# Turning the gates behind the scores in a gated linear attention kernel

## The chip, the cores and the metric

The kernel runs on one core of one Trainium2 chip. The metric is device time in microseconds (us), from inputs in HBM to the output in HBM; lower is better. Engines are named as the profile names them: PE is TensorE (PEld its weight loads), DVE is VectorE, ACT is ScalarE, POOL is GpSimd, SP is SyncE, which here only issues DMAs.

## The reference, cut to what matters

Attention with a gated state, then a routed expert network, then a dense network. Only the first part is touched by the change:

```
q, k, v, f_logit: (4, 8, 768, 48)          # batch, heads, sequence, head dimension
f = 1 / (1 + exp(-f_logit))
for t in range(S):
    state = f[:, :, t, :, None] * state + einsum('bhd,bhe->bhde', k[:, :, t], v[:, :, t])
    y[:, :, t] = einsum('bhd,bhde->bhe', q[:, :, t], state)
x = y as (3072, 384)
x = expert network of x: 8 experts, 384 -> 1024 -> 384, 384 tokens each, chosen by sorted logits
out = (h * clip(h + 3, 0, 6) / 6) @ w_out,  h = x @ w_in,  384 -> 2048 -> 384
```

## The kernel before

Each engine has its own program, and semaphores order them. Attention is cut into 24 units: 6 tiles of 128 positions times 4 batches (NT = 24, B = 4). A unit has all 8 heads of one batch in one tile, as 4 pairs of heads. `units` (L443) writes units 0 to 3 out, puts 4 to 19 into a loop whose body holds four units (so n is a register expression there), and writes 20 to 23 out. The first unit of a loop body is therefore 4, 8, 12 or 16.

The inputs come with positions on the partitions, and the products need head dimensions there, so TensorE turns them against the identity: `turn_f`, `turn_k`, `turn_q` (L1394 on), each four transposes of 128x128 recorded at L1392. It works ahead: in unit n it turns f and k of unit n + 2 and q of unit n + 1. The rest of a unit on TensorE, in this order: the scores (L1448, k_sc by q_sc, 16 passes in tiles of 64x128), the turn of the scaled k called kn (L1459, in all but the last four units), the turns of k and q, `turn_y` of the unit before (L1431, 128x128), the state's part of y (L1475, 64x64), the products of k and v for the state (L1484, 128x64), and the values (L1491, 128x48). The last unit's turn_y stands behind all units.

What the turn of f starts is a chain over three engines:
- ScalarE: `exp(n + 2)` (L792, e_x from the turned f; waits for f_turned), then den (L796).
- VectorE: `products(n + 2)` (L999), a scan over den that gives grow. It waits for den_done, then for ln_done, error_done (up to 2n - 1) and k_scaled.
- ScalarE: `decays(n + 2)`, lnr (L802) and guess (L806).
- GpSimd: `refine(n + 2)` of its unit n: error (L688), error again (L691), decay (L696), then last_decay (L683), and behind it w_low of the weight chunk (L708), a subtraction in which both inputs lie in SBUF.
- VectorE: `scale_k(n + 2)` (L1005) needs grow; `scale_q(n + 1)` (L1010) needs decay of n + 1.

VectorE's order in a unit is the mask of the scores (L1048, two instructions), the scan, scale_k, scale_q, kv_sum (L1067), the logits (L1015), the state (L1073). ScalarE's is exp, den, the copy of kn (L836), the copies of x (L817, L820), lnr, guess, the cast of a weight chunk (L827), the copy of y (L845). The scores of unit n + 1 need q_sc of n + 1, which is VectorE's scale_q in unit n.

SP issues the loads of f, k, q and v four units ahead into four buffers each (the load of f(n) waits until f(n - 4) is turned), and with each unit one store of x and one load of a weight chunk, in one queue.

Unit 0 has seven matmuls of filling (`busy`) behind its turn of f, before the scores.

Of the kernel before, what the change touches and what calls it, by code (L numbers as in the profile page):

```python
# [15 lines left out]
B, H, S, D = 4, 8, 768, 48  # L16
# [41 lines left out]
def build(nc, q, k, v, f, wg, w1, w2, wi, wo, out):  # L58
    ctx = ExitStack()
    with ctx:  # L60
# [392 lines left out]
        def start_of(n):  # L453

            return n if isinstance(n, int) else NT

        def more_state(tt):

            return not isinstance(tt, int) or tt < TT - 1
# [925 lines left out]
        def _(pe):  # L1385
# [3 lines left out]
            def turn(n, tt, b, src, dst, here, done):  # L1389
                pe.wait_ge(here[b], 16 * (tt + 1))  # L1390
                for g in range(PAIRS):
                    last = pe.transpose(dst[:, P * g:P * g + P], src[:, b, 2 * g:2 * g + 2, :].rearrange("p a b -> p (a b)"), ident[:, :])  # L1392
                last.then_inc(done, 1)

            def turn_f(n, tt, b):
                if start_of(n) >= 1:
                    pe.wait_ge(exp_done, n)
                turn(n, tt, b, f_in, fT_ps, loaded_f, f_turned)

            def turn_k(n, tt, b):  # L1400
                if start_of(n) >= 1:
                    pe.wait_ge(k_scaled, n)
                turn(n, tt, b, k_in, kT_ps, loaded_k, k_turned)

            def turn_q(n, tt, b):
                if start_of(n) >= 1:
                    pe.wait_ge(q_scaled, n)
                turn(n, tt, b, q_in, qT_ps, loaded_q, q_turned)

            def busy(count):  # L1410
                for i in range(count):
                    pe.matmul(p4[:, P * (i % 4):P * (i % 4) + P], ident[:, :], ident[:, :], start=True, stop=True)
# [9 lines left out]
            def turn_y(n, i):  # L1422
                pe.wait_ge(yT_copied, n + 1)
                if start_of(n) >= 1:
                    pe.wait_ge(x_copied, n)
                else:
                    pe.wait_ge(loaded_wg, 48)
                    pe.wait_ge(turn_made, 2)
                pe.sem_inc(passed, 1)
                for g in range(PAIRS):  # L1430
                    last = pe.matmul(x_ps[:, g, :], yT[:, i, P * g:P * g + P], turn_gate[:, g, :], start=True, stop=True)  # L1431
                last.then_inc(x_ready, 1)

            def unit(n, tt, b, more):
                i = b % 2
                if more:
                    turn_f(n + 2, tt + b // 2, (b + 2) % B)
                if isinstance(n, int) and n == 0:
                    busy(BUSY[2])
                pe.wait_ge(q_scaled, n + 1)  # L1440
                pe.wait_ge(k_scaled, n + 1)
                if start_of(n) >= 1:
                    pe.wait_ge(masked, n)
                pe.sem_inc(passed, 1)
                for g in range(PAIRS):
                    for j in range(2):
                        r = slice(HALF * j, HALF * j + HALF)
                        last = pe.matmul(a_ps[j][:, P * g:P * g + P], k_sc[r, i, P * g:P * g + P], q_sc[r, i, P * g:P * g + P],  # L1448
                                         start=True, stop=True)
                last.then_inc(a_ready, 1)  # L1450
                if not more_state(tt) and b == B - 1:
                    pe.wait_ge(steep_rows, 1)
                    pe.wait_ge(exp_done, NT)
                    pe.matmul(p0[:, 0:1], ones[:, :], steep_sum[:, :], start=True, stop=True).then_inc(steep_summed, 1)
                if more_state(tt):
                    if start_of(n) >= 1:
                        pe.wait_ge(kv_added, n)
                    for g in range(PAIRS):
                        last = pe.transpose(kn_ps[:, P * g:P * g + P], k_sc[:, i, P * g:P * g + P], ident[:, :])  # L1459
                    last.then_inc(kn_ready, 1)  # L1460
                if more:
                    turn_k(n + 2, tt + b // 2, (b + 2) % B)
                if more or b < B - 1:
                    turn_q(n + 1, tt + (b + 1) // B, (b + 1) % B)
                if start_of(n) >= 1:
                    turn_y(n - 1, 1 - i)
                if start_of(n) >= B:
                    pe.wait_ge(state_done, n - B + 1)
                if start_of(n) >= 1:
                    pe.wait_ge(yT_copied, n)  # L1470
                pe.sem_inc(passed, 1)
                for h in range(H):
                    g, j = h // 2, h % 2
                    r = slice(HALF * j, HALF * j + HALF)
                    last = pe.matmul(yT_ps[r, P * g:P * g + P], state[r, b, g, :], q_sc[r, i, P * g:P * g + P],  # L1475
                                     start=(g == 0), stop=False, skip_group_check=True)
                last.then_inc(y_init, 1)
                pe.wait_ge(loaded_v[b], 16 * (tt + 1))
                if more_state(tt):
                    pe.wait_ge(kn_copied, n + 1)  # L1480
                    pe.sem_inc(passed, 1)
                    for h in range(H):
                        g, j = h // 2, h % 2
                        last = pe.matmul(kv_ps[HALF * j:HALF * j + HALF, g, :], kn[:, P * g + HALF * j:P * g + HALF * j + HALF],  # L1484
                                         v_in[:, b, h, :], start=True, stop=True)
                    last.then_inc(kv_ready, 1)
                pe.wait_ge(masked, n + 1)
                pe.sem_inc(passed, 1)
                for h in range(H):
                    g, j = h // 2, h % 2  # L1490
                    last = pe.matmul(yT_ps[HALF * j:HALF * j + D, P * g:P * g + P], v_in[:, b, h, :], a_sb[:, i, j, g, :],  # L1491
                                     start=False, stop=(g == PAIRS - 1), skip_group_check=True)
                last.then_inc(y_ready, 1)
            units(pe, unit)
            go = steep_flag(pe)
            turn_y(NT - 1, (B - 1) % 2)
# [305 lines left out]
```

## Time and profile before

| | us |
|---|---|
| median of 3 runs | 829.54 (829.25 to 831.32) |
| the profiled execution | 828.84 |
| its span | 827.1 |
| PE busy in the span | 798.6 (97%) |
| DVE, ACT, POOL busy | 358.1, 318.1, 328.3 |
| mean granted clock of TensorE | 0.992 of full speed |

The first 169 us are attention, then comes the routing to about 207 us, then the experts and the dense network to the end. In slices of a fortieth of the span (20.7 us) PE is at 9 tenths or more from the second to the seventh, and DVE at 8, so that stage has little slack on either; behind it, in the experts' stage, PE alone is full. Below, rows in order of time have the start in us, the duration in us, the engine, the line, what is written from what, the count of instructions, and in brackets how long the engine was idle before and who ended that.

### The profile page before, as it was taken

The numbers are of one execution on the slowest core, as the hardware profiler recorded it, in microseconds if no ns is written. First come the engines' busy times: TensorE is split into PE (matmuls) and PEld (weight loads), VectorE is DVE, ScalarE is ACT, GpSimd is POOL, SyncE is SP. The second block draws the span as 40 slices with busy tenths as digits, with TensorE's granted clock in tenths as the row PEclk, the third lists the DMA queues.
The fourth block names the chain that finished last, engine by engine and source line by source line (L and its number), as shares of the span: only waits on it lengthen the run. The fifth ranks groups of instructions, "written<-read, shape, count | busy, mean of one in ns | idle before, by whom it ended". The sixth has DMA issues, their size and how long they took to land.

```text
span 827.1 us, 15012 instructions
## 1 busy us (share of the span) xinstructions
PE 798.6 (97%) x5785; PEld 762.4 (92%) x5785; DVE 358.1 (43%) x653; ACT 318.1 (38%) x626; POOL 328.3 (40%) x247
## 2 busy tenths in 40 slices
PE   7899999986999999999999999999999999999996
PEld 6788888844999999999999999999999999999996
DVE  7888888655234314422431343144224323431332
ACT  4776667512233314322332333134324323332332
POOL 3778888746144115322602440254216124401001
PEclk9999999998999999999999999999999999999999
DMA  9999999542113012210221040122102210200000
GB/s 153 202 192 184 213 190 191 109 172 97 39 26 128 15 43 77 77 58 0 76 76 57 3 149 0 57 76 76 47 10 76 76 57 0 76 0 29 1 0 29
DMA packets 126801, 64.97 MB, mean 79 GB/s; under 512 B 102448, under 2 KB 119856, under 8 KB 126768
## 3 DMA queue, kind: packets, MB, share of 16 engines
q1 hardware_dynamic: 123696, 55.09, 30.4%
q0 software_dynamic: 3072, 9.44, 3.6%
q8 instruction: 21, 0.34, 0.2%
q14 instruction: 12, 0.10, 0.0%
HBM read 55.07 MB, written 9.44 MB: 78 GB/s over the span
## 4 chain that ended last, share of the span: by engine, by line
PE 90%; DVE 3%; SPq 3%; DMA 2%; issue 1%; ACT 1%; POOL 0%; POOLq 0%; DVEq 0%; ACTq 0%
PE psum L1666 24%; PE psum L1668 24%; PE psum L1667 24%; PE psum L1392 3%; PE psum L1448 3%; PE psum L1475 2%; PE psum L1431 2%; PE psum L1491 2%; SPq L530 2%; PE psum L1459 1%; PE psum L1484 1%; PE psum L1677 1%; PE psum L1575 1%; DMA f_in<-in_f_logit_dram 1%; DMA raw<-in_moe_w_in_dram 1%
## 5 line engine op out<-in xcount | busy, mean ns | idle before, releaser
L1374 DVE SCALAR_TENSOR_TENSOR psum<-rg,psum 128x384 f32<-128x384 f32 x128 | 71.9, 562 | 155.1 <-ACT rg L945 155.1
L945 ACT ACTIVATE rg<-psum,three 128x384 f32<-128x384 f32 x128 | 74.4, 581 | 153.0 <-PE psum L1668 153.0
L1666 PE MATMUL psum<-yh,w_high 128*128 128x384 f32 x384 | 130.6, 340 | 0.8
L1666 PE MATMUL psum<-w_high,gh 128*128 128x384 f32 x384 | 128.4, 334 | 0.3 <-DVE gl L1377 0.3
L1668 PE MATMUL psum<-yh,w_low 128*128 128x384 f32 x384 | 128.4, 334 | 0.0
L1667 PE MATMUL psum<-yl,w_high 128*128 128x384 f32 x384 | 128.4, 334 | 0.0
L1668 PE MATMUL psum<-w_high,gl 128*128 128x384 f32 x384 | 128.3, 334 | 0.0
L1667 PE MATMUL psum<-w_low,gh 128*128 128x384 f32 x384 | 128.3, 334 | 0.0
L781 POOL DMA_INDIRECT out_dram<-ys,ids x24 | 24.0, 999 | 251.2 <-ACT ys L960 246.4
L1364 DVE SCALAR_TENSOR_TENSOR hl<-psum,hh 128x384 fp32r<-128x384 f32 x64 | 35.7, 558 | 164.9 <-ACT hh L935 158.3
L1377 DVE SCALAR_TENSOR_TENSOR gl<-psum,gh 128x384 fp32r<-128x384 f32 x128 | 71.4, 558 | 72.3 <-ACT gh L949 72.3
L949 ACT ACTIVATE gh<-psum 128x384 fp32r<-128x384 f32 x128 | 62.9, 491 | 81.4 <-DVE psum L1374 81.4
L935 ACT ACTIVATE hh<-psum 128x384 fp32r<-128x384 f32 x64 | 31.5, 492 | 144.9 <-PE psum L1668 144.3
L723 POOL CAST w1h<-raw 128x3072 fp32r<-128x3072 f32 (+1 forms) x13 | 22.9, 1764 | 138.6 <-PE psum L1668 128.3
L1666 PEld LDWEIGHTS psum<-yh,w_high 128*128 128x128 f32 x384 | 72.1, 188 | 4.3 <-DVE yl L1368 3.4
L1666 PEld LDWEIGHTS psum<-w_high,gh 128*128 128x128 f32 x384 | 72.1, 188 | 0.6 <-DVE gl L1377 0.6
L1667 PEld LDWEIGHTS psum<-yl,w_high 128*128 128x128 f32 x384 | 72.2, 188 | 0.0
L1668 PEld LDWEIGHTS psum<-yh,w_low 128*128 128x128 f32 x384 | 72.1, 188 | 0.0
L1667 PEld LDWEIGHTS psum<-w_low,gh 128*128 128x128 f32 x384 | 72.1, 188 | 0.0
L1668 PEld LDWEIGHTS psum<-w_high,gl 128*128 128x128 f32 x384 | 72.1, 188 | 0.0
L1666 PE MATMUL psum<-xh,w1h 128*128 128x384 f32 (+2 forms) x198 | 65.8, 332 | 0.5 <-DVE xl L1358 0.2
L1668 PE MATMUL psum<-xh,w1l 128*128 128x384 f32 (+2 forms) x198 | 65.6, 331 | 0.0
(194 smaller groups left out, 1504.7 us busy)
## 6 DMA issues: line engine op xcount, KB each, us to landing
raw<-in_moe_w_dram SPq DMA_DIRECT2D x15, 1536.0 KB, 6.5
f_in<-in_f_logit_dram SPq DMA_DIRECT2D x24, 192.0 KB, 4.7
k_in<-in_k_dram SPq DMA_DIRECT2D x24, 192.0 KB, 5.1
q_in<-in_q_dram SPq DMA_DIRECT2D x24, 192.0 KB, 5.3
v_in<-in_v_dram SPq DMA_DIRECT2D x24, 192.0 KB, 4.7
x_rows<-x_nat SPq DMA_DIRECT2D x24, 192.0 KB, 4.1
raw<-in_moe_w_in_dram SPq DMA_DIRECT2D x12, 256.0 KB, 4.3
raw<-in_moe_w_out_dram SPq DMA_DIRECT2D x12, 256.0 KB, 3.2
```

Source lines behind the costliest of these rows:

```text
L781: pool.indirect_dma_start(out=out[:, :], out_offset=bass.IndirectOffsetOnAxis(ap=ids[:, 3 * e + t:3 * e + t + 1].bitcast(U32), axis=0), in ...
L935: act.activation(hh[:, j % 2, :], banks[j % 2][:, 0:CAP], ACT.Relu).then_inc(hh_done, 1)
L945: act.activation(rg[:, j % 2, :], banks[j % 3][:, 0:CAP], ACT.Relu, bias=three[:, 0:1]).then_inc(r_done, 1)
L949: act.mul(gh[:, j % 3, :], banks[j % 3][:, 0:CAP], 1.0 / 6.0).then_inc(gh_done, 1)
L1364: dve.scalar_tensor_tensor(out=hl[:, j % 2, :], in0=banks[j % 2][:, 0:CAP], scalar=0.0, in1=hh[:, j % 2, :].bitcast(F32), op0=ALU.max, op1 ...
L1374: dve.scalar_tensor_tensor(out=bank, in0=rg[:, j % 2, :], scalar=6.0, in1=bank, op0=ALU.min, op1=ALU.mult).then_inc(gg_done, 1)
L1377: dve.scalar_tensor_tensor(out=gl[:, j % 3, :], in0=bank, scalar=1.0 / 6.0, in1=gh[:, j % 3, :].bitcast(F32), op0=ALU.mult, op1=ALU.subtra ...
L1392: last = pe.transpose(dst[:, P * g:P * g + P], src[:, b, 2 * g:2 * g + 2, :].rearrange("p a b -> p (a b)"), ident[:, :])
L1448: last = pe.matmul(a_ps[j][:, P * g:P * g + P], k_sc[r, i, P * g:P * g + P], q_sc[r, i, P * g:P * g + P], start=True, stop=True)
L1666: pe.matmul(bank, high, rhs_high, start=start, stop=False)
L1667: pe.matmul(bank, high, rhs_low, start=False, stop=False)
L1668: return pe.matmul(bank, low, rhs_high, start=False, stop=stop)
```

## The change

In unit n, for all n but 0, the turn of f of unit n + 2 no longer stands at the head of the unit, between the values of unit n - 1 and the scores of unit n; it stands right behind the scores, ahead of the turns of kn, k and q. In unit 0 (`opening`) it stays where it is, with the filling behind it. The waits go with it: turn_f waits for exp_done of the unit before and for the load of f.

```
             def unit(n, tt, b, more):
                 i = b % 2
-                if more:
-                    turn_f(n + 2, tt + b // 2, (b + 2) % B)
-                if isinstance(n, int) and n == 0:
+                opening = isinstance(n, int) and n == 0
+                if opening:
+                    turn_f(2, 0, 2)
                     busy(BUSY[2])
                 pe.wait_ge(q_scaled, n + 1)
                 pe.wait_ge(k_scaled, n + 1)
...
                 last.then_inc(a_ready, 1)
+                if more and not opening:
+                    turn_f(n + 2, tt + b // 2, (b + 2) % B)
                 if not more_state(tt) and b == B - 1:
```

## Rows read from the trace of the kernel before

**Rows 1.** Busy time of each engine in a stretch; the columns stand in the first line.
```profile
core 0: us, PE busy (x) PEld busy (x) DVE busy (x) ACT busy (x) POOL busy (x), PEclk, DMA share, GB/s
100.00:120.00 20.00, 20.00 (x270) 17.67 (x268) 16.56 (x25) 14.22 (x28) 16.74 (x16) 1.00 1.18 193
```

**Rows 2.** Weight loads of TensorE in order of time, unit 7 and the next f.
```profile
60.53 0.42 PEld L1392 LDWEIGHTS psum<-ident,f_in 128*128 128x128 f32 x4 [0.18 <-issue]
61.12 0.97 PEld L1448 LDWEIGHTS psum<-q_sc,k_sc 64*128 64x128 f32 x16 [0.17 <-issue]
62.21 0.42 PEld L1459 LDWEIGHTS psum<-ident,k_sc 128*128 128x128 f32 x4
62.60 0.47 PEld L1392 LDWEIGHTS psum<-ident,k_in 128*128 128x128 f32 x4
63.03 0.47 PEld L1392 LDWEIGHTS psum<-ident,q_in 128*128 128x128 f32 x4
...
65.56 0.55 PEld L1484 LDWEIGHTS psum<-v_in,kn 128*64 128x64 f32 x16 [0.17 <-issue]
66.02 0.83 PEld L1491 LDWEIGHTS psum<-a_sb,v_in 128*48 128x48 f32 x16
67.04 0.42 PEld L1392 LDWEIGHTS psum<-ident,f_in 128*128 128x128 f32 x4 [0.19 <-issue]
```

**Rows 3.** ScalarE in order of time, unit 7.
```profile
61.23 0.60 ACT L792 ACTIVATE e_x<-psum 128x512 f32<-128x512 f32 x1
61.86 0.63 ACT L796 ACTIVATE den<-e_x 128x512 f32<-128x512 f32 x1
...
65.10 0.64 ACT L802 ACTIVATE lnr<-grow 128x512 f32<-128x512 f32 x1
```

**Rows 4.** VectorE in order of time, unit 7.
```profile
62.33 1.29 DVE L1048 TENSOR_TENSOR a_sb<-psum,causal 128x512 f32<-128x512 f32 x2 [0.95 <-PE psum L1448]
63.53 1.25 DVE L999 TENSOR_TENSOR_SCAN grow<-den,cap 128x516 f32<-128x516 f32 x1
```

**Rows 5.** GpSimd in order of time, unit 7.
```profile
63.68 2.18 POOL L708 TENSOR_TENSOR w_low<-raw,w_high 128x512 f32 x1
66.49 1.18 POOL L688 TENSOR_TENSOR error<-grow,guess 128x512 f32<-128x512 f32 x1 [0.63 <-ACT guess L806]
```

**Rows 6.** Weight loads of TensorE, the turn of f in unit 9.
```profile
73.91 0.42 PEld L1392 LDWEIGHTS psum<-ident,f_in 128*128 128x128 f32 x4 [0.55 <-issue]
```

**Rows 7.** VectorE's q_sc in unit 1 and TensorE's scores in unit 2.
```profile
27.74 0.68 DVE L1010 TENSOR_TENSOR q_sc<-psum,decay 128x512 f32<-128x512 f32 x1
...
28.54 1.00 PEld L1448 LDWEIGHTS psum<-q_sc,k_sc 64*128 64x128 f32 x16 [0.60 <-issue]
```

**Rows 8.** The turns of f in units 20 and 21, and q_sc between.
```profile
145.53 0.42 PEld L1392 LDWEIGHTS psum<-ident,f_in 128*128 128x128 f32 x4 [0.18 <-issue]
...
150.47 0.68 DVE L1010 TENSOR_TENSOR q_sc<-psum,decay 128x512 f32<-128x512 f32 x1
...
151.13 0.42 PEld L1392 LDWEIGHTS psum<-ident,f_in 128*128 128x128 f32 x4 [0.18 <-issue]
```

**Rows 9.** Scores, mask, scan and w_low in order of time, unit 8.
```profile
67.63 1.16 PE L1448 MATMUL psum<-q_sc,k_sc 64*128 64x128 f32 x16
...
68.93 1.29 DVE L1048 TENSOR_TENSOR a_sb<-psum,causal 128x512 f32<-128x512 f32 x2 [1.04 <-PE psum L1448]
...
70.13 1.22 DVE L999 TENSOR_TENSOR_SCAN grow<-den,cap 128x516 f32<-128x516 f32 x1
70.18 2.25 POOL L708 TENSOR_TENSOR w_low<-raw,w_high 128x512 f32 x1
```

**Rows 10.** w_low, scan and q_sc of unit 4, scores of unit 5.
```profile
44.02 1.27 POOL L708 TENSOR_TENSOR w_low<-raw,w_high 128x512 fp32r<-128x512 f32 x1
...
44.11 2.27 DVE L999 TENSOR_TENSOR_SCAN grow<-den,cap 128x516 f32<-128x516 f32 x1
...
47.12 0.68 DVE L1010 TENSOR_TENSOR q_sc<-psum,decay 128x512 f32<-128x512 f32 x1
...
48.10 0.64 PEld L1448 LDWEIGHTS psum<-q_sc,k_sc 64*128 64x128 f32 x10 [0.17 <-issue]
```

## The prediction

> **What bounds the kernel now.** First the busy time by stretch: in attention, where the change is, TensorE is busy 20.00 of 20 us at a granted clock of 1.00; the reader is to see that VectorE (16.6 us) and GpSimd (16.7 us) are near it too [rows 1]. Then TensorE's weight loads in order of time, for one unit (unit 7; units 0 to 23 are the 24 pairs of tile and batch). I count from the start of f's turn: f 0, scores 0.59, kn 1.68, k 2.07, q 2.50, ..., values 5.49, next f 6.51 [rows 2]. So a unit lasts 6.51 us. Loads of one tile shape follow each other without a gap (kn to k 0.39, k to q 0.43), but where the shape changes there is one: 66.85 to 67.04 before f (0.19), 60.95 to 61.12 before the scores (0.17), 62.09 to 62.21 before kn (0.12). TensorE waits for nobody here; it pays for changes of shape.
>
> Last the other engines in the same unit, since the turn of f(n+2) heads a chain: ScalarE's exp starts 0.70 after f's first load, den ends 1.26 after exp's start, VectorE's scan, then lnr, guess, and GpSimd's error [rows 3 to 5]. Today the scan waits for the mask of the scores (1.80) and starts at 3.00, while den is ready at 1.96.
>
> **The change part by part.** Durations are from the profiled execution: 828.84 us, span 827.10, so 1.74 us lie around the span; the median of the runs is 829.54, 0.70 above it. I sum against 828.84 and add the 0.70 at the end.
>
> (a) Removed: one change of shape per unit. No matmul goes or comes, only the order: values, scores, f, kn. f costs 0.59 today (0.42 of loads and the gap 0.17) and 0.44 between scores and kn (as k and q do). Gain 0.15 per unit, a unit of 6.36. The gap between values and scores is a pair of shapes that the trace doesn't have; the nearest rows bound it by 0.12 and 0.19 [rows 2], I take 0.19, which is what follows the values today; by the other end there is 0.07 more per unit. Units 3 to 19: 17 x 0.15 = 2.55 us gained.
>
> (b) Unit 9 waits today before f's turn, for the load of f: idle 0.55 instead of 0.19, so 0.36 [rows 6]. The turn is asked for 1.09 later in the unit now, so this wait goes: 0.36 gained. The load of k is next in line there; it isn't late in sum, since by (c) and (f) the units before are not ahead of today's.
>
> (c) Unit 2 loses. Today f's turn lies under the wait of its scores for q_sc, which ends at 28.42; the scores start at 28.54 after an idle of 0.60 [rows 7]. Behind the scores f has no such cover: 0.44 lost. Unit 1 is held by the first weight chunk further on and neither gains nor loses; unit 0 keeps its order.
>
> (d) Units 20 and 21 (5.60 us, without kn) gain nothing: q_sc of the next unit is done at 151.15, 5.62 into unit 20 [rows 8], the scores could start 0.12 later, at 5.74, and the unit would otherwise be down to 5.45. I take 0.15 lost for the two together.
>
> (e) SP's load of f into a buffer waits for the turn of four units back, so 1.09 of lateness holds nothing behind it (k, q, v, the store and the weight chunk on the same queue). The waits of turn_f (exp_done, loaded_f) now stand ahead of kn, k, q; exp_done is of the unit before, the load is there. kn's copy on ScalarE moves behind den to 3.05, its reader on TensorE is at 4.88: covered.
>
> (f) The chain of f. f's first load moves to 1.09, exp to 1.79, den ends at 3.05. Today's scan starts at 3.00; the mask, 0.59 earlier, no longer holds it. Outside the loop the scan would follow at 3.08. In the loop's body products(n) waits for den_done first, and then come the register arithmetic for 2n-1 and further waits: I count two steps between that wait and the scan, and at the first unit of a body (4, 8, 12, 16) one more there and one ahead of exp. What a step behind a wait costs shows in the mask: the scores' matmuls take 1.16, and the mask starts 0.05 us after the last in unit 7 (62.28 to 62.33), 0.14 in unit 8 (68.79 to 68.93), the first of a body [rows 2, 4, 9]: 0.09. It is at least nothing and, by these rows, at most 0.09; I take 0.085. The scan then starts at 3.08 + 2 x 0.085 = 3.25, and 2 steps later, at 3.42, in the first units of a body.
>
> That lateness alone is harmless: scan 1.22, k_sc and q_sc done 1.42 after it (46.38 to 47.80 in unit 4), and 0.12 to the scores: 6.01, under 6.36. What matters is GpSimd's w_low, which starts at 3.15 [rows 5]. VectorE and GpSimd shut each other out: in unit 8 the scan starts 0.05 ahead of w_low, takes 1.22, and w_low 2.25 [rows 9]; in unit 4 it starts 0.09 behind w_low (44.11 against 44.02) and takes 2.27, until 1.09 after w_low's end [rows 10]. There q_sc is ready at 47.80 and the next scores start at 48.10, undisturbed, because f's turn (0.59) stands before them. This is the cover that the change takes away.
> Where is w_low then? It hangs on the scan itself: lnr 0.03 after its end, error 1.39 after lnr's start, w_low 3.69 after error's start (66.49 to 70.18) [rows 3, 5, 9] (the 0.03 is the pause between exp's end and den's start in rows 3, an estimate for this step). So 3.25 + 1.22 + 0.03 + 1.39 + 3.69 - 6.36 = 3.22: in most units the scan comes 0.03 behind w_low, in the first of a body 0.20 to 0.28 behind.
> The first of a body surely loses: w_low ends at 3.15 + 1.27 = 4.42 or 4.49, the scan 1.09 later, scores of the next unit at 5.51 or 5.58 + 1.42 + 0.12 = 7.05 or 7.12 instead of 6.36: 0.69 once and 0.76 three times, 2.97 us.
> At 0.03 it is open: the rows have 0.05 ahead (won) and 0.09 behind (lost). Shut out, w_low ends 1.08 beyond the scan's end (64.78 to 65.86 in unit 7, 71.35 to 72.43 in unit 8) and takes 1.27 alone, so 0.19 of it was over when it was stopped; the scan ends 1.09 beyond w_low and takes 1.22 alone, so 0.13. By that w_low asks some 0.06 later after its start than the scan does, and a scan 0.03 behind is still first. I take it as won.
>
> Sum: -2.55 - 0.36 + 0.44 + 0.15 + 2.97 = +0.65. What comes behind attention shifts with it. 828.84 + 0.65 = 829.5 against the profiled time, 830.2 beside the median.
>
> **The rivals.**
> A, nothing collides: the steps behind the wait are free, the scan starts at 3.08 everywhere, ahead of w_low. Then only (a) to (d): -2.32: 826.5 by the profile, 827.2 beside the median. For it: every such step may run ahead while the wait lasts. Against it: unit 8's mask.
> B, the forecast: four collisions, 830.2.
> C, the slower side: the scan loses also at 0.03. The place is the start of every scan against w_low; it decides from the point where a scan that starts behind w_low is shut out. After a collision GpSimd is a unit's 0.7 late and the next scan is free; the one after collides again. So every second unit from 4 to 18, 8 x 0.75 = 6.0, less 2.32: +3.7, 833.2 beside the median. For it: unit 4 at 0.09. Against it: the durations above.
> The Trainium skill (SBUF — State Buffer, "SBUF: two separate sides") calls the port pair that VectorE and GpSimd share an exclusive lock: whichever instruction starts first has it for the whole instruction, and a VectorE operation with two inputs in SBUF takes part. Read by the start times of the rows that rule gives C; units 4 and 8 agree with it, and no row has a scan 0.03 behind.
> D, the change doesn't do what it says: the new pair of shapes costs 0.34 or the neighbours gain nothing, so (a) is nil: B becomes +3.2, 832.7. Nothing in the rows speaks for it; three pairs of shapes all lie at 0.12 to 0.19.
>
> **How the numbers follow.** Chances: B 0.45, C 0.32, A 0.13, D and mixtures (some more or fewer collisions) 0.10. This kernel can tell 0.3%, 2.5 us, from no change. A lies at -0.28%, half of it counts as faster, with some of the mixtures and the unknown gap: faster 0.12. C and D are slower, the edge of B too: slower 0.36. Same 0.52. The range goes from 827.2, the middle of A, to 833.8, which is C with 0.6 for the steps' cost; about 0.06 is left out below and 0.10 above. B's own range is 828.8 to 831.7: down by the other end of (a)'s gap (20 x 0.07 = 1.4), up by two more collisions (0.75 each).
>
> **What would show it.** Right in (a): loads of scores 0.19 behind the values, f without a gap before kn, units of 6.36 us where nothing waits. Right in (f): den to scan about 0.2 us in the body, scans of some 2.1 us in units 4, 8, 12, 16 with the scores of the unit after them waiting for q_sc 0.7 us, and scans of 1.22 elsewhere. C would show scans over 2 us in every second unit. A would show no wait of the scores for q_sc between units 4 and 19, and TensorE's attention 2.3 us shorter. Wrong altogether would be a unit longer than 6.36 for another reason: kn's copy late, a load of k late at units 8 to 11, or the mask behind the state's update.

## The result: slower by half a per cent, by the rival with the shut-out scans

After the change the median is 833.34 us (832.31 to 833.87, 6 runs), before it 829.39 us (828.23 to 831.32, 6 runs, the same chip): ratio 1.0048, 95% interval 1.0038 to 1.0057. The forecast was 830.2 with a range of 827.2 to 833.8; the time is in the range, but it is that of rival C (833.2), to which the prediction gave a chance of 0.32 against 0.45 for its own case. What it called likeliest, no change beyond 0.3% (0.52), did not come; the time lies in the range because the range was drawn wide enough for C.

The page of the kernel after: busy time of each engine over the whole span.

```profile
span 832.1 us, 15012 instructions
PE 796.9 (96%) x5785; PEld 763.9 (92%) x5785; DVE 362.8 (44%) x653; ACT 317.3 (38%) x626; POOL 321.0 (39%) x247
```

The same stretch of attention as [rows 1], by engine:

```profile
100.00:120.00 20.00, 18.57 (x261) 16.75 (x260) 17.50 (x24) 13.10 (x27) 13.52 (x14) 1.00 1.24 192
```

TensorE is busy 18.57 of 20 us where it was 20.00, at the same granted clock of 1.00: something now makes it wait. The view of TensorE's waits over 0 to 175 us (us in total, times, longest) names it:

```profile
PE psum L1448 <- DVE q_sc L1010: 8.5, 13, 1.3
PE psum L1392 <- DVE cap L973: 4.9, 1, 4.9
PE psum L1392 <- DMA f_in<-in_f_logit_dram: 0.2, 1, 0.2
```

The scores (L1448) wait for q_sc 13 times, 8.5 us. Unit 6 shows how a unit goes now. TensorE's weight loads (answering to [rows 2]) from its scores to those of unit 7, each with its start, its duration and, in brackets, the idle time ahead of it:

```profile
56.04 0.97 PEld L1448 LDWEIGHTS psum<-q_sc,k_sc 64*128 64x128 f32 x16 [0.19 <-issue]
57.13 0.42 PEld L1392 LDWEIGHTS psum<-ident,f_in 128*128 128x128 f32 x4
57.52 0.47 PEld L1461 LDWEIGHTS psum<-ident,k_sc 128*128 128x128 f32 x4
57.95 0.47 PEld L1392 LDWEIGHTS psum<-ident,k_in 128*128 128x128 f32 x4
...
61.38 0.83 PEld L1493 LDWEIGHTS psum<-a_sb,v_in 128*48 128x48 f32 x16
63.15 1.00 PEld L1448 LDWEIGHTS psum<-q_sc,k_sc 64*128 64x128 f32 x16 [0.94 <-issue]
```

VectorE in the same unit (answering to [rows 4, 10]):

```profile
57.25 1.29 DVE L1048 TENSOR_TENSOR a_sb<-psum,causal 128x512 f32<-128x512 f32 x2 [0.29 <-PE psum L1448]
59.28 2.33 DVE L999 TENSOR_TENSOR_SCAN grow<-den,cap 128x516 f32<-128x516 f32 x1 [0.75 <-ACT den L796]
61.75 0.69 DVE L1005 TENSOR_TENSOR k_sc<-psum,grow 128x512 f32<-128x512 f32 x1
62.35 0.68 DVE L1010 TENSOR_TENSOR q_sc<-psum,decay 128x512 f32<-128x512 f32 x1
```

And GpSimd (answering to [rows 5]):

```profile
57.64 1.28 POOL L696 TENSOR_TENSOR decay<-guess,error 128x512 f32<-128x512 f32 x1
59.09 0.19 POOL L683 COPY last_decay<-decay 128x4 f32 x1 [0.17 <-POOL decay L696]
59.26 1.26 POOL L708 TENSOR_TENSOR w_low<-raw,w_high 128x512 f32 x1
63.02 1.19 POOL L688 TENSOR_TENSOR error<-grow,guess 128x512 f32<-128x512 f32 x1 [2.49 <-ACT guess L806]
```

The scan starts 0.02 behind w_low and takes 2.33 us where it needs 1.23; it ends 1.09 after w_low's end (60.52), q_sc ends at 63.03, and the scores start at 63.15 after an idle of 0.94, of which 0.19 is the change of shape and 0.75 the wait. The next unit's scan stands where it always does (66.43, 3.28 behind its scores) and is free, because everything on GpSimd hangs on the late scan and w_low comes late with it:

```profile
66.43 1.23 DVE L999 TENSOR_TENSOR_SCAN grow<-den,cap 128x516 f32<-128x516 f32 x1 [0.76 <-ACT den L796]
```

```profile
67.61 1.28 POOL L708 TENSOR_TENSOR w_low<-raw,w_high 128x512 f32 x1
```

In unit 8, the first of a body, the scan is shut out again:

```profile
72.97 2.15 DVE L999 TENSOR_TENSOR_SCAN grow<-den,cap 128x516 f32<-128x516 f32 x1 [0.83 <-ACT den L796]
```

```profile
72.76 1.27 POOL L708 TENSOR_TENSOR w_low<-raw,w_high 128x512 f32 x1
```

The scans of units 3, 4, 6, 8, 10, 12, 14, 16 and 18 take 2.15 to 2.35 us, those of the others from unit 2 on 1.23 to 1.25 (unit 1's takes 2.03, before 1.97). From unit 6 on a pair of units lasts 6.36 + 7.14 us, against 2 x 6.51.

**Where the time came from.** Counting from the end of the unit before (f's turn before, the scores after): unit 3 began at 34.49 and begins at 35.41, unit 20 at 145.53 and at 150.56, unit 23 at 161.74 and at 166.87. So +0.92 by unit 3, +4.11 in units 3 to 19, +0.10 in units 20 to 22. Units 3 to 19 now last 115.15 = 17 x 6.36 + 7.03 us of waits. The profiled execution after is the slowest of its six (833.87; before 828.84), so its +5.0 is more than the +3.95 of the medians; 0.24 of it stands already at unit 0's scores (13.63 against 13.39), ahead of anything that the change moves.

### The profile page after: what moved, and what is told of

Read it like the earlier page. It is cut to its first block, busy times and chain, and to the rows that moved or that the text cites. A ratio compares the mean times of both kernels' runs of the same rounds, so it can differ in the third digit from the quotient of the medians.

```text
span 832.1 us, 15012 instructions
## 1 busy us (share of the span) xinstructions
PE 796.9 (96%) x5785; PEld 763.9 (92%) x5785; DVE 362.8 (44%) x653; ACT 317.3 (38%) x626; POOL 321.0 (39%) x247
## 4 chain that ended last, share of the span: by engine, by line
PE 85%; DVE 6%; ACT 3%; issue 2%; SPq 2%; DMA 1%; POOL 0%; DVEq 0%; POOLq 0%; ACTq 0%
PE psum L1668 24%; PE psum L1670 24%; PE psum L1669 24%; DVE grow L999 3%; PE psum L1448 3%; PE psum L1392 2%; SPq L530 2%; PE psum L1477 1%; PE psum L1431 1%; PE psum L1493 1%; DVE q_sc L1010 1%; ACT den L796 1%; ACT e_x L792 1%; PE psum L1679 1%; PE psum L1577 1%
```

## The experiments

All were timed against the kernel before on the same chip, whose median was 828.6 to 829.4 us. "New" is the changed kernel, "old" the one before. w_low is needed after attention only.

**1 and 2. w_low taken away, new and old.** Both leave out GpSimd's subtraction (w_low is zero, so the products with it are).

```diff
-                pool.tensor_tensor(chunk_at(w_low, n), raw..., ALU.subtract).then_inc(chunk_split, 1)
+                pool.sem_inc(chunk_split, 1)
+            pool.memset(w_low[:, :].bitcast(F32), 0.0)      # once, ahead of the units
             keep_last(0, 0)
```

> The new order, with GpSimd's 24 subtractions into w_low left out (w_low is set to zero once before unit 2, so the low part of the dense network's weights is missing). Theory L (every second scan starts 0.03 us behind w_low, is shut out until w_low has ended, and the scores of the next unit wait for q_sc): with no w_low no scan takes over 1.3 us between units 4 and 19, units are 6.36 us, and the kernel is 1.5 to 2.3 us faster than before, 827.1 to 827.9. Rival S (the scan is late because the gates are turned 1.09 us later, and this lateness alone costs, with or without GpSimd): no change against the new order, 833.3. Rival G (putting f between scores and kn saves no change of tile shape): 829.4 or slower with all scans at 1.2 us.

> The old order, with the same subtractions left out. It is the control of the run before: does w_low cost anything in the old order? Theory L: no, because a scan that is shut out there ends under the cover of f's turn: 829.4, within 0.4 us of before; one long scan (unit 4) goes and TensorE's loads keep their times. If w_low slowed the old order too, this would be 1 us or more faster, and part of what the run before gains would not be the order's.

Measured: new 833.08 (ratio 1.0048, 1.0034 to 1.0062), old 835.34 (1.0074, 1.0060 to 1.0087). The totals are spoiled by the one memset I added. VectorE and GpSimd of the old order without w_low, in unit 0:

```profile
8.81 0.69 DVE L1005 TENSOR_TENSOR k_sc<-psum,grow 128x512 f32<-128x512 f32 x1
10.06 0.69 DVE L1019 TENSOR_TENSOR error<-grow,guess 128x512 f32<-128x512 f32 x1 [0.56 <-ACT guess L806]
10.79 8.62 DVE L1021 TENSOR_SCALAR error<-error 128x512 f32<-128x512 f32 x1
```

```profile
8.79 10.34 POOL L698 MEMSET w_low<- 128x12288 f32 x1
```

The memset holds a VectorE instruction of 0.43 us (before, at 10.77) for 8.62. What stands is the inside: in both kernels all scans of the loop take 1.22 to 1.25, no scores wait in units 3 to 19, and units 3 to 19 last 108.12 us in the new order, 110.68 in the old: 17 x 6.36 and 17 x 6.51.

**3. The waits in another order** (new). products(n) and exp(n) wait for the late semaphore last.

```diff
             def products(n):
-                dve.wait_ge(den_done, n + 1)
                 if start_of(n) >= 1:
                     ...
                     dve.wait_ge(k_scaled, n)
+                dve.wait_ge(den_done, n + 1)
```

> The new order, all work kept, only the order of waits changed: products(n) waits for ln_done, error_done and k_scaled first and for den_done last, exp(n) for den_done first and f_turned last, so no register step stands between the late signal and the instruction. Theory L with the steps: the scan starts 3.08 after the head of the unit instead of 3.25 (3.42 in the first unit of a loop body), 0.06 or more ahead of w_low, and wins from unit 6 on; units 3 to 5 may still collide (about 1.5 us). 827.5 to 829.3. Rival T (the 0.17 is not the steps but ScalarE or the semaphore): scan still at 3.25, every second one over 2 us, 833.3.

Measured: 828.91, ratio 0.9997 (0.9988 to 1.0006). The scan of unit 7 and w_low beside it:

```profile
64.54 1.23 DVE L999 TENSOR_TENSOR_SCAN grow<-den,cap 128x516 f32<-128x516 f32 x1 [0.58 <-ACT den L796]
```

```profile
64.61 2.24 POOL L708 TENSOR_TENSOR w_low<-raw,w_high 128x512 f32 x1
```

The unit's scores stand at 61.46, so the scan is at 3.08 (3.25 in the new kernel) and first; the units last 6.36. So the steps behind the wait made the scan late, some 0.085 each, and without them the new order loses no scan of the body. In units 3 and 20 of the new kernel, which are written out with the same waits but constants in place of the register arithmetic, the scan stands at 3.08 too, which points to the register arithmetic and not to the waits themselves. Behind unit 2 one collision is left, in unit 20, with its price:

```profile
147.37 2.26 DVE L999 TENSOR_TENSOR_SCAN grow<-den,cap 128x516 f32<-128x516 f32 x1 [0.74 <-ACT den L796]
```

```profile
147.28 1.27 POOL L708 TENSOR_TENSOR w_low<-raw,w_high 128x512 f32 x1
```

```profile
151.14 1.00 PEld L1448 LDWEIGHTS psum<-q_sc,k_sc 64*128 64x128 f32 x16 [1.73 <-issue]
```

In that shorter unit the scores wait 1.54 beyond the 0.19 of the shape.

**4. w_low behind the scan** (new).

```diff
                 pool.wait_ge(chunk_high, n + 1)
+                if more and (not isinstance(n, int) or n + 3 < NT):
+                    pool.wait_ge(grow_done, n + 4)
                 pool.tensor_tensor(chunk_at(w_low, n), raw...
```

> The new order, all work kept, but w_low of unit n waits on GpSimd for grow_done of the scan that it would meet (unit n + 3), so the scan always comes first and w_low runs behind it, from 4.6 to 5.9 of the unit; error of the next unit starts at 5.9 anyway. Theory L: all scans at 1.2 us, units of 6.36 us, 1.5 to 2.3 us faster than before, 827.1 to 827.9, like the run without w_low. If GpSimd's own time were what binds, w_low's later end would delay error, decay and q_sc: 833 or slower. Rival S: 833.3.

Measured: 827.13, ratio 0.9973 (0.9963 to 0.9983). VectorE and GpSimd in unit 13 of this kernel:

```profile
102.87 1.23 DVE L1001 TENSOR_TENSOR_SCAN grow<-den,cap 128x516 f32<-128x516 f32 x1 [0.75 <-ACT den L798]
```

```profile
103.03 1.06 POOL L683 COPY last_decay<-decay 128x4 f32 x1 [0.17 <-POOL decay L696]
104.31 1.29 POOL L710 TENSOR_TENSOR w_low<-raw,w_high 128x512 f32 x1 [0.21 <-DVE grow L1001]
```

The scan is as late as in the new kernel (3.25, and 3.42 in the first unit of a body), takes 1.23 throughout the loop, and the loss of the new kernel is gone. It now meets only the copy last_decay, which starts 0.16 behind it and takes 1.06 instead of 0.19. What makes the new kernel slow is the collision, not the lateness. TensorE's waits (0 to 175 us) show what is left:

```profile
PE psum L1394 <- DMA f_in<-in_f_logit_dram: 1.9, 3, 0.7
PE psum L1450 <- DVE q_sc L1012: 1.3, 4, 0.5
```

The loads of f are late in units 7 and 8 (0.51 and 0.72 of waiting; the scans of these two units stand at 3.79 and 4.20 for it); unit 20 begins at 144.15, 1.4 ahead of before, and without these two waits it would be 2.6 ahead. The shorter unit doesn't by itself bring these waits: between 30 and 160 us TensorE waits for f not at all in experiments 1 and 3, whose units are 6.36 as well, and 1.1, 1.7 and 1.9 us in experiments 6, 10 and 11, whose units are 6.51. Their cause is open.

**5 and 6. GpSimd's place in the loop left empty, new and old.** w_low of the loop is left out, and zeroed piecewise in the units that are written out.

```diff
-                pool.tensor_tensor(chunk_at(w_low, n), raw..., ALU.subtract).then_inc(chunk_split, 1)
+                if isinstance(n, int):
+                    pool.memset(w_low[:, at:at + 1536].bitcast(F32), 0.0).then_inc(chunk_split, 1)
+                else:
+                    pool.sem_inc(chunk_split, 1)
```

> The first pair of runs without w_low was spoiled at the start: the one memset of 10.3 us that zeroed w_low stopped a VectorE instruction of unit 0 for 8 us. Here, in the new order, w_low's subtractions are left out in the loop's units 4 to 19 with nothing in their place, and in the eight units written out a memset of 1536 columns stands for each (the low part of the dense network's weights is missing). Theory L: no scan over 1.3 us and no wait of the scores in units 4 to 19, units of 6.36 us, loads of f or k may be waited for around unit 8 by up to 1 us in sum: 827.0 to 828.2. Rival S (lateness alone): 833.3.

> The same in the old order, the control. Theory L: w_low costs nothing there: units of 6.51 us, 829.0 to 829.8, and the pair differs by 1 to 2.5 us, which is the order's own gain. If w_low cost the old order something, 828 or less.

Measured: new 827.11 (0.9977, 0.9967 to 0.9987), old 829.02 (0.9998, 0.9988 to 1.0008). Without collisions the order is worth 1.9 us by the medians, and taking w_low out of the old order is worth nothing.

**7. A collision forced on the old order, first try.** The copy last_decay is left out (the flag that it feeds is then constant), so that w_low starts earlier.

```diff
-                pool.tensor_copy(last_decay[...], by_pair(decay[...])[...]).then_inc(low_done, 1)
+                pool.sem_inc(low_done, 1)
```

> The old order, made to collide: GpSimd's copy into last_decay is left out in all units (last_decay is set to 1 once, so the test for steep gates always says no), so w_low starts some 0.17 us earlier in its unit, about 2.98 after its head against the scan's 3.00. Theory L with the cover: many scans, every second one or more, are shut out and take over 2 us as in the new order, q_sc is ready at about 6.7 and the scores, behind f's turn at 7.1, don't wait: 829.0 to 829.8, as before. If a collision costs by itself, whatever the order on TensorE, 8 of them at 0.75 give 833 to 836.

Measured: 829.36, ratio 1.0006 (0.9994 to 1.0019). The setup missed: from unit 6 on every scan stayed first, by a hair. In the loop only those of units 4 and 5 were shut out (2.25 and 1.85 us), as in the kernel before (2.27 and 1.86), so no collision was added. The scan and w_low of unit 9:

```profile
78.51 1.22 DVE L1000 TENSOR_TENSOR_SCAN grow<-den,cap 128x516 f32<-128x516 f32 x1
```

```profile
78.53 2.28 POOL L709 TENSOR_TENSOR w_low<-raw,w_high 128x512 f32 x1 [0.35 <-POOL decay L695]
```

It gives the other side of the question that the prediction left open: 0.02 ahead of w_low a scan is first; 0.02 behind it (59.28 against 59.26 above) it is not, nor in unit 4 of the new kernel, where both are recorded at 45.76.

**8. Experiment 4 with f at the head of units 0, 1, 2, 20 and 21.**

```diff
+                at_head = isinstance(n, int) and n in (0, 1, 2, 20, 21)
+                if at_head:
+                    turn_f(n + 2, tt + b // 2, (b + 2) % B)
...
-                if more and not opening:
+                if more and not at_head:
```

> The new order with w_low behind the scan (827.1 measured), and with the turn of f back at the head of units 1, 2, 20 and 21, where the new place gains nothing: in unit 2 it lies under the wait for q_sc, in 20 and 21 the scores of the next unit wait for q_sc. Theory: 0.4 us at unit 2, of which the loads around units 7 and 8 take back most or all, and 0.1 to 0.3 us at 20 and 21: 826.5 to 827.1. If q_sc isn't what binds at 20 and 21, 827.4 or slower.

Measured: 826.53, ratio 0.9968 (0.9957 to 0.9979), by the ratio 2.7 us below before (by the medians of that chip, 828.64 and 826.53, 2.1) and the fastest of all; its interval and that of experiment 4 overlap, so the part of the five units is not shown.

**9. A collision forced on the old order, second try.** A memset of nothing's use ahead of the scan.

```diff
+                if not isinstance(n, int):
+                    dve.memset(pause[:, :], 0.0)
                 dve.tensor_tensor_scan(...
```

> The old order (f between values and scores) with a memset of 208 numbers per partition (about 0.27 us, nothing uses it) on VectorE ahead of each scan of the loop's body. It puts the scan at about 3.27 after a unit's f turn while w_low stays at 3.14, so that the scan is shut out in every second unit, as in the new order. Theory 'cover': a shut-out scan costs the old order nothing, since it ends 1.09 after w_low, q_sc is ready at 6.2 and the next scores start at 7.10 behind f's turn: seven to nine scans of about 2.2 us, no wait of scores for q_sc, and the time of the kernel before, 828.9 to 830.2. Rival 'collisions cost by themselves' (0.75 us each, whatever the order): 834.5 to 836.5. If the scans stay at 1.22, the setup failed and nothing follows.

Measured: 828.72, ratio 1.0005 (0.9994 to 1.0016). The setup missed again. VectorE, then GpSimd, in unit 8:

```profile
70.43 0.23 DVE L1001 MEMSET pause<- 128x208 f32 x1
70.58 1.17 DVE L1002 TENSOR_TENSOR_SCAN grow<-den,cap 128x516 f32<-128x516 f32 x1
```

```profile
70.41 2.41 POOL L709 TENSOR_TENSOR w_low<-raw,w_high 128x512 f32 x1
```

The scan starts 0.17 behind w_low and still runs undisturbed, while w_low is held. It has no wait of its own to sit out and follows the memset without a gap. In unit 4 the same pair comes later against w_low, and the scan loses:

```profile
44.41 0.23 DVE L1001 MEMSET pause<- 128x208 f32 x1
44.56 2.05 DVE L1002 TENSOR_TENSOR_SCAN grow<-den,cap 128x516 f32<-128x516 f32 x1
```

```profile
44.26 1.27 POOL L709 TENSOR_TENSOR w_low<-raw,w_high 128x512 fp32r<-128x512 f32 x1
```

The memset takes 0.23 in all 16 units, here too, where w_low had started 0.15 before it: it is never held itself. So it isn't shown that the memset shuts w_low out; a scan that stands ready behind it may also ask earlier than its recorded start. The rows do not part these two.

**10. The edit of experiment 4 on the old order.**

```diff
+                if more and (not isinstance(n, int) or n + 3 < NT):
+                    pool.wait_ge(grow_done, n + 4)
```

> The old order with the one edit that gained in the new order: w_low waits for the scan of unit n+3. Theory 'cover': in the old order no scan's lateness reaches TensorE, so taking the collisions away gains nothing: 829.0 to 829.9, units still 6.51 us. Rival 'the edit gains by itself, whatever the order' (its gain in the new order was 6 us): 827.5 or less.

Measured: 829.63, ratio 1.0004 (0.9994 to 1.0014). Its units last 6.51 where no load is late. The edit has no gain of its own: its 6 us in the new order are the collisions' price there.

**11. A collision forced on the old order, third try.** The scan waits for VectorE's own mask, and its other waits follow.

```diff
             def products(n):
+                if not isinstance(n, int):
+                    dve.wait_ge(masked, n - 1)
                 dve.wait_ge(den_done, n + 1)
```

> The old order; in the loop's body the scan waits for the end of VectorE's own mask, and its other waits follow that one. By the rows a step behind a wait costs about 0.085 us and a VectorE instruction that waits for the one before starts 0.04 behind its end instead of 0.09 ahead: the scan should start at 3.2 to 3.35 after a unit's f turn, w_low at 3.14 as before, with nothing of VectorE's in between. Theory 'the late scan is shut out, and the old order covers it': every second scan of the body takes 2.1 to 2.3 us (seven to nine of them), the scores behind it wait for nobody (q_sc ready at 6.2, scores at 7.1), units stay 6.51, the time is that of the kernel before, 828.9 to 830.2. Rival 'a collision costs 0.75 us whatever the order': 834.5 to 836.5. If the scans stay at 1.2 us, the setup failed again.

Measured: 829.28, ratio 1.0006 (0.9996 to 1.0015). This time it collides. VectorE, GpSimd and TensorE's weight loads around the end of unit 15:

```profile
118.38 2.20 DVE L1001 TENSOR_TENSOR_SCAN grow<-den,cap 128x516 f32<-128x516 f32 x1 [0.35 <-DVE a_sb L1050]
120.71 0.69 DVE L1007 TENSOR_TENSOR k_sc<-psum,grow 128x512 f32<-128x512 f32 x1
121.32 0.68 DVE L1012 TENSOR_TENSOR q_sc<-psum,decay 128x512 f32<-128x512 f32 x1
```

```profile
118.23 1.26 POOL L708 TENSOR_TENSOR w_low<-raw,w_high 128x512 f32 x1
```

```profile
121.45 0.42 PEld L1394 LDWEIGHTS psum<-ident,f_in 128*128 128x128 f32 x4 [0.18 <-issue]
122.12 1.00 PEld L1450 LDWEIGHTS psum<-q_sc,k_sc 64*128 64x128 f32 x16 [0.25 <-issue]
```

Eleven scans of the body take over 1.4 us, six of them 1.82 to 2.20. The scores behind them idle 0.17 to 0.25, of which 0.17 is the shape; the units behind them last 6.62 at most where no load is late, and the time is that of the kernel before. In the new kernel the same 2.2 us cost 0.75 a time. The cover named in the prediction, f's turn between the values and the scores, is real. I had expected every second scan to collide and a start at 3.2 to 3.35; it was about every third in full, and the start was 3.44, later still and yet covered.

## Why the prediction was right or wrong

- **(a), right.** 17 x 6.36 and 17 x 6.51 in experiments 1 and 2; the scores stand 0.19 behind the values (56.04) and kn's load follows f's without a gap (57.13 to 57.52). The pair of shapes that no row had costs the 0.19 taken for it, so rival D is out. The Trainium skill (TensorEngine Tiling (Array Packing), "Key Properties") says that a change of tiling mode drains TensorE; the 0.15 that goes with one change fewer agrees. The move gained its 2.55.
- **(b), right by its sign, its reason not shown.** The wait for f in unit 9 went. But it is also missing in experiments 2 and 9, where f stands at the head as before, and waits for f of 0.4 to 1.2 us in sum come in experiments 4, 5 and 8. The prediction took for a trait of the order what differs from run to run (see experiment 4).
- **(c), too small.** Unit 3 begins 0.92 later instead of 0.44. Of this 0.25 is the late start from unit 0, which reaches unit 2 through q_sc (ready at 28.67 against 28.42) and isn't the change's. The other 0.67 is the 0.44 and 0.23 in unit 2's scores, whose first matmul starts 0.26 behind its load (before 0.03); why is open. Experiment 8 doesn't tell this part apart.
- **(d), right:** +0.10 for 0.15. **(e), right for kn:** its reader is not late (kn's copy ends at 103.15 in experiment 4, its reader on TensorE starts at 104.51); for the loads see (b).
- **(f), the step that failed.** The mechanism and its places were right: the scan stands at 3.25 and, in first units of a body, at 3.42; w_low at 3.22; a collision gives a scan of 2.15 to 2.35 and, from unit 6 on, costs 0.75 in the unit after it (forecast 0.69 to 0.76). What failed is the sentence "a scan 0.03 behind is still first. I take it as won." It rested on durations: w_low "asks some 0.06 later after its start". The runs have 0.02 ahead won (experiment 7) and 0.02 behind lost (unit 6 and every second unit after it). So nine scans were shut out instead of four (four of the five more, in units 6, 10, 14 and 18, by this 0.02; the fifth, unit 3's, was 0.07 behind, since w_low stands at 3.01 there and the prediction had not looked at it), and 7.03 us of waits stand where the sum had 2.97. Rival A fell by the same starts; experiment 3 shows what A needed.
- **The sum.** 7.03 - 2.55 - 0.36 = 4.12 for units 3 to 19 (measured 4.11), + 0.92 + 0.10 = 5.1 in the profiled executions. C had counted eight collisions and 0.44 in (c). So a few hundredths of a start decided 4 us. The prediction quoted the rule that gave C (SBUF — State Buffer, "SBUF: two separate sides", in the Trainium skill: the pair belongs to whichever starts first) and weighed it below its own difference of two durations; where the scan had waited for den, the runs agree with the rule; experiment 9's scan behind a memset is no such case.

## What to carry to other kernels

A move that takes a change of tile shape away on the bounding engine is worth its 0.15 us a time only if the chain it delays still ends in time; look for what used to lie over that chain's worst case, not its usual one. Two instructions on VectorE and GpSimd whose starts fall within 0.1 us are a race that one register step can turn: order them by a semaphore (experiment 4: 6 us back, and 2.3 us below before) instead of reckoning the hundredths. Put the wait for the late semaphore last among an instruction's waits; here that alone moved the scan by 0.17 and was worth 4.4 us against the changed kernel (833.34 to 828.91).

## What the runs showed of the hardware that was not expected

- Beside GpSimd's memset of 10.34 us a VectorE instruction with one input in SBUF took 8.62 us (alone 0.43), and the one with two inputs in SBUF 0.69 as always (experiment 2). The Trainium skill (SBUF — State Buffer, "SBUF: two separate sides") says that two SBUF inputs count only against a GpSimd operation that reads SBUF, and a 2-port mode counts always; these rows agree with the first, and with the second if the held instruction ran in such a mode, which no row shows.
- The recorded start alone doesn't decide. A scan right behind a memset kept w_low out (w_low 2.41) although it started 0.17 after it (experiment 9), while a scan that had waited for den and started 0.02 behind w_low lost. The memset itself took 0.23 even where w_low was already running. What makes the difference is open.
- Register arithmetic behind a wait was not free, also where the wait before it was long (0.75 us): the scan stands at 3.25 instead of 3.08 for what I count as two steps, at 3.42 for four, some 0.085 a step, and at 3.08 in written-out units with the same waits.
